# Attention with two mixture layers on one core: block means of the last units turned a slot sooner, and the order of step 1 around its normalisation changed

## The chip, the core and the metric

The kernel runs on one core of one Trainium2 chip. The metric is the device time of one execution in microseconds. Before the change three executions took 823.92, 826.63 and 828.28 us; the median is 826.63 us.

## What is computed

The program has three stages in a row, all in 32-bit floating point. Two sequences of 768 tokens with 8 heads of 64 features go through an attention in which a query sees the 31 keys around it and 24 block summaries (the maximum of a block's 32 keys, the mean of its 32 values). The result, 1536 tokens of 512 features, goes through a mixture of four experts and then through one wide layer.

```python
def _attn_ref(q, k, v):
    k_sum = k.reshape(B, H, nb, block, D).max(axis=3)
    v_sum = v.reshape(B, H, nb, block, D).mean(axis=3)
    scores_l = scale * np.matmul(q, k.transpose(0, 1, 3, 2))      # masked to |i - j| < 16
    scores_s = scale * np.einsum('bhsd,bhnd->bhsn', q, k_sum) + np.log(block)
    a = softmax(concatenate([scores_l_m, scores_s]))
    return np.matmul(a, concatenate([v, v_sum], axis=2))

def _moe_ref(x, domain_probs, w1, w2):
    p = domain_probs / (domain_probs.sum(-1, keepdims=True) + 1e-09)
    for e in range(4):
        out += p[:, e:e + 1] * (np.maximum(x @ w1[e], 0.0) @ w2[e])

def _moe2_ref(x, w_in, w_out):
    h = x @ w_in
    return (h * (1.0 / (1.0 + np.exp(-1.702 * h)))) @ w_out
```

## The kernel before

**Attention in slots.** The attention is cut into 8 units (one sequence, two heads) of 3 groups k. Units 0 to 3, groups 0 to 11, run in a software pipeline of 18 slots in which each engine does one stage of several groups: TensorE the scores of group slot-1, VectorE the mask, ScalarE the exponentials, VectorE the inverted sums (`invert_sums`), GpSimd the normalisation (`normalize`), TensorE the transposes, VectorE or ScalarE the copy of the transposed weights, TensorE the values, ScalarE the copy into `xa` (`take_x`). Units 4 to 7 are spread over the steps behind.

**Block means and maxima.** For each unit VectorE sums the blocks of values (`value_sums`, `v_sum`), TensorE turns the sums (`turn_value_sums`, line L1628), ScalarE scales them (`value_means`, L958) and GpSimd spreads them over the value windows (`spread_value_means`, L708). VectorE takes the maxima of the keys (`key_maxima`, L1271) and GpSimd spreads them (`spread_key_maxima`, L690). Unit 4 (named `KT` in the code) has its maxima taken at the end of the slots and its values summed in step 1.

**Steps.** The mixtures are 48 steps g. A step holds one pair of blocks of hidden features; its first matrix product is made by seven half-size products P1 to P7 (a Strassen scheme, order P1, P2, P5, P6, P7, P4, P3), and the second one by eight pieces `down(g, t)`. Each number is split in a high and a low part, so that a product is three matmuls (L1651, L1652, L1653). Step 0 has four plain tiles instead (`first_tile`), which start as soon as the blocks of `xa` are split: ScalarE makes the high parts (`high_moved`), VectorE the low parts (`low_moved`, L1348).

**Weights.** The weights of a step come by one 1 MB transfer into `stage[g % 2]`. GpSimd makes four sums (`sum_weights`, L719 to L725), the low parts of what came (`low_raw`, L730) and of the sums (`low_sums`, L736), and those of the second matrix (`low_down`, L742; for step 0 `low_first`, L752 and L758). ScalarE makes the high parts (`high_raw`, L982; `high_sums`; `high_down`). On step g TensorE weaves the products of step g with `down(g - 1, t)`. Behind product P6 ScalarE keeps a copy of a bank (`keep(g, 1)`, L1024), for which P7 waits.

**Orders.** All orders are written out by hand, one instruction stream for each engine, and every engine works its own in order. SyncE issues all transfers from one list. In its list the values of unit 5 stand behind a wait for unit 4's `value_sums`, since both use the same buffer, and behind them come the value windows of unit 5, two stores of split weights of step 1 and the load of `stage` for step 3:

```python
def load_value_columns(u):
    if u >= KT:
        sp.wait_ge(vsum_done, u)
    sp.dma_start(v_cols[values_at(u)][:], v_t[u, :, :])
```

Of the kernel before, what the change touches and what calls it, by code (L numbers as in the profile page):

```python
# [19 lines left out]
KT = DM // P  # L20
# [7 lines left out]
B_GROUPS = KT * GROUPS  # L28
# [37 lines left out]


B12, T2 = 7, 3
MADE_0 = (0, B12, 6, 2, 1, 3, 4, 5)

READY_0 = {"C12": 1, "C22": 2, "C11": 3, "C21": 4}

# [47 lines left out]
def attention_moe_ffn(nc, consts, q_t, k_w, v_t, v_w, probs, weights, p_rows, split, out):  # L120
    ctx = ExitStack()
    with ctx:
# [174 lines left out]
        def values_due(slot, lag):  # L297


            return [u for u in range(KT) if slot - lag == GROUPS * u + L_SUM + (u > 0)]  # L300
# [381 lines left out]
        def _(pool):  # L682
# [44 lines left out]
            def low_raw(g):  # L727

                pool.wait_ge(rawhi_done, own(g))
                nc.gpsimd.tensor_tensor(wu_lo[:, g % 2, 0:RAW], stage[:, g % 2, 0:RAW],  # L730
                                        wu_hi[:, g % 2, 0:RAW].bitcast(F32), ALU.subtract).then_inc(rawlo_done, 1)
# [13 lines left out]
            def low_first(n):  # L745

                half = slice(RAW // 2 * (n % 2), RAW // 2 * (n % 2 + 1))
                if n < 2:
                    pool.wait_ge(rawhi_done, 1)
                    if n == 1:  # L750
                        pool.wait_ge(rawlo_first, 1)
                    nc.gpsimd.tensor_tensor(wu_lo[:, 0, half], stage[:, 0, half], wu_hi[:, 0, half].bitcast(F32),  # L752
                                            ALU.subtract).then_inc(rawlo_first if n == 0 else rawlo_done, 1)
                else:
                    pool.wait_ge(dnhi_done, 2)
                    if n == 3:
                        pool.wait_ge(dnlo_first, 1)
                    nc.gpsimd.tensor_tensor(wd_lo[:, 0, half], stage[:, 0, 4 * BW:][:, half],  # L758
                                            wd_hi[:, 0, half].bitcast(F32),
                                            ALU.subtract).then_inc(dnlo_first if n == 2 else dnlo_done, 1)  # L760
# [74 lines left out]
            for slot in range(SLOTS):  # L835
                for k in group(slot, L_NORM):
                    normalize(k)
                for u in keys_due(slot):
                    spread_key_maxima(u)
                for u in values_due(slot, 2):  # L840
                    if u:
                        spread_value_means(u, norm_done, slot - L_NORM + 1)
                    else:
                        spread_value_means(u, kwin_done, 2)
                if slot in (11, 12):
                    low_first(slot - 11)

            for g in range(STEPS):
                ph, part = preparing(g)
# [15 lines left out]
                if more:  # L865
                    sum_weights(g + 1)
                    if g == 0:
                        spread_key_maxima(KT)
                    low_raw(g + 1)
                for k in step_group(g):  # L870
                    normalize(k)
                if ph == 2 and part == 0:

                    sum_moved(ph, 1)
                    low_down(g)
                    low_moved(ph, 0)
                    low_moved(ph, 2)
                    sum_moved(ph, 2)
                    low_moved(ph, 1)
                    low_down(g + 1)  # L880
                    continue
# [60 lines left out]
        def _(act):  # L942
# [24 lines left out]
            def take_x(k):  # L967

                act.wait_ge(pv_done, k + 1)
                nc.scalar.activation(columns(k), x_bank(k)[:, 0:GT * QT], ACT.Copy).then_inc(x_done, 1)  # L970
# [119 lines left out]
            for slot in range(SLOTS):  # L1090
                for k in group(slot, L_X):
                    take_x(k)
                for k in group(slot, L_EXP):
                    exponent(k)
                for k in group(slot, L_TRANS):
                    if on_act(k):
                        copy_prob_t(k)
                for u in values_due(slot, 1):
                    value_means(u)
                if slot == 10:  # L1100
                    high_raw(0)
                if slot == 12:
                    high_moved(0, 0)
                if slot == 13:
                    high_moved(0, B12)
                if slot == 14:
                    high_down(0, 0)
                    high_down(0, 1)
                if slot == 16:
                    high_moved(0, 6)  # L1110
                    high_moved(0, 2)
            high_moved(0, 1)
            high_raw(1)
            high_sums(1)
            high_hidden(0, "C12")
# [148 lines left out]
        def _(dve):  # L1264
# [165 lines left out]
            for slot in range(SLOTS):  # L1430
                if slot == 0:
                    key_maxima(0)
                for k in group(slot, L_EXP):
                    mask_scores(k)
                for k in group(slot, L_NORM):
                    invert_sums(k)
                for k in group(slot, L_TRANS):
                    if not on_act(k):
                        copy_prob_t(k)
                for u in keys_due(slot):  # L1440
                    key_maxima(u)
                for u in values_due(slot, 0):
                    value_sums(u)
                if slot == 1:
                    normalize_weights()
                if slot == 13:
                    low_moved(0)
                if slot == 14:
                    low_moved(B12)
                    sum_first(1)  # L1450
                if slot == 15:
                    key_maxima(KT)
            low_moved(6)
            low_moved(2)
            low_moved(1)
            gate(0, "C12")
            gate(0, "C22")
            low_hidden(0, "C12")
# [11 lines left out]
            for g in range(1, STEPS):  # L1470
                if g == 1:

                    add_c11(1)
                    mask_scores(B_GROUPS)
                    gate(1, "C11")
                    take_y(0, 0)
                    value_sums(KT)
                    take_y(0, 1)
                    low_hidden(1, "C11")
                    invert_sums(B_GROUPS)  # L1480
                    take_y(0, 2)
                    low_moved(5)
                    take_y(0, 3)
                elif second(g):
                    if paired(g - 3):
                        take_product(g - 3, "P4", 1)
# [102 lines left out]
        def _(pe):  # L1589
# [170 lines left out]
            for slot in range(SLOTS):  # L1760
                for k in group(slot, L_SCORE):
                    scores(k)
                for k in group(slot, L_TRANS):
                    transpose(k)
                for k in group(slot, L_VAL):
                    values(k)
                for u in values_due(slot, 1):
                    turn_value_sums(u)
            pe.wait_ge(rawlo_done, 1)
            pe.wait_ge(vmean_done, KT)  # L1770
            pe.wait_ge(xlo_dve, low_parts(0, 0))
# [20 lines left out]
            product(1, "P7")  # L1792
            down(0, 2)
            down(0, 3)
            turn_value_sums(KT)
            down(0, 4)
            down(0, 5)
            transpose(B_GROUPS)
            product(1, "P4")
            down(0, 6)  # L1800
# [113 lines left out]
```

## Time and profile before

| | |
|---|---|
| median of three executions | 826.63 us |
| lowest, highest | 823.92, 828.28 us |
| profiled execution, its own time | 824.39 us |
| its span (first to last instruction) | 822.2 us |
| granted TensorE clock, mean share | 0.998 |
| TensorE busy | 798.7 us, 97% |
| VectorE, ScalarE, GpSimd busy | 69%, 52%, 71% |

The profiled execution lies 2.24 us under the median; 2.2 us of its time lie outside the span. TensorE is nearly always busy, so the table says that only its gaps and its own work make the time; where those gaps are, the rows below tell.

### The profile page before, as it was taken

To read this page: it belongs to the slowest core of one execution; us is meant where nothing else is said; L and a number is where in the kernel's file an instruction comes from. 1 tells how busy PE (TensorE), PEld (TensorE's weight loads), DVE (VectorE), ACT (ScalarE), POOL (GpSimd) and SP (SyncE) were. 2 spreads that over 40 slices of the span, in tenths; PEclk is the share of its full clock that TensorE was granted. 3 is DMA by queue.
4 is the path that set the end of the run, shared out by engine and by line. 5 is a ranking of instruction groups with operands and counts; after the bars stand their busy time and mean duration, and the time that the engine had idled before them with its cause. 6 is when DMAs were issued, how large, how long until landed. Compare 5 with 4: busy or idle time off the path is not lost.

```text
span 822.2 us, 14168 instructions
## 1 busy us (share of the span) xinstructions
PE 798.7 (97%) x4894; PEld 779.6 (95%) x4894; DVE 568.6 (69%) x1194; ACT 427.8 (52%) x943; POOL 580.8 (71%) x406
## 2 busy tenths in 40 slices
PE   5889999999999999999999999999999999999997
PEld 4778999999999999999999999999999999999997
DVE  5888656666665566687877877665666665677777
ACT  3865445445445454546545544434456553656663
POOL 3697765655666699678778685777488873588794
PEclk9999999999999999999999999999999999999999
DMA  9959547375444354446245343343544445373412
GB/s 265 285 122 338 214 196 235 141 262 216 159 179 175 141 214 161 171 155 232 104 184 198 122 198 142 142 189 143 217 160 187 175 172 205 104 293 143 165 66 77
DMA packets 39957, 148.92 MB, mean 181 GB/s; under 512 B 16208, under 2 KB 17360, under 8 KB 36688
## 3 DMA queue, kind: packets, MB, share of 16 engines
q1 hardware_dynamic: 39888, 148.03, 49.9%
q8 instruction: 39, 0.64, 0.3%
q14 instruction: 30, 0.25, 0.1%
HBM read 100.81 MB, written 47.21 MB: 180 GB/s over the span
## 4 chain that ended last, share of the span: by engine, by line
PE 76%; POOL 10%; issue 5%; ACT 4%; DVE 3%; DMA 1%; SPq 0%; ACTq 0%; DVEq 0%; POOLq 0%
PE bank L1651 25%; PE bank L1653 24%; PE bank L1652 24%; POOL wd_lo L809 2%; POOL h_raw L832 2%; POOL t_raw L832 2%; PE bank L1606 2%; ACT prob L949 1%; PE bank L1617 1%; PE bank L1643 1%; DMA v_cols<-v_t 1%; ACT xb_first_hi L1050 1%; POOL wu_lo L730 1%; POOL wd_lo L742 1%; ACT xb_last_hi L1074 0%
## 5 line engine op out<-in xcount | busy, mean ns | idle before, releaser
L1358 DVE TENSOR_TENSOR xa<-bank,xa 128x384 f32<-128x384 f32 x208 | 115.8, 556 | 136.7 <-PE bank L1653 133.9
L1651 PE MATMUL bank<-h_hi,wd_hi 128*128 128x384 f32 x448 | 150.5, 336 | 0.3 <-DVE xa L1356 0.2
L1653 PE MATMUL bank<-h_lo,wd_hi 128*128 128x384 f32 x448 | 149.8, 334 | 0.0
L1652 PE MATMUL bank<-h_hi,wd_lo 128*128 128x384 f32 x448 | 149.7, 334 | 0.0
L1040 ACT ACTIVATE h_hi<-bank 128x384 fp32r<-128x384 f32 x112 | 55.1, 492 | 136.9 <-DVE bank L1415 113.5
L742 POOL TENSOR_TENSOR wd_lo<-stage,wd_hi 128x1024 fp32r<-128x1024 f32 x27 | 65.2, 2413 | 82.9 <-ACT wd_hi L997 82.8
L809 POOL TENSOR_TENSOR wd_lo<-stage,wd_hi 128x512 fp32r<-128x512 f32 x60 | 85.9, 1437 | 40.2 <-ACT wd_hi L1087 39.5
L1651 PE MATMUL bank<-xb_other_hi,wu_hi 128*128 128x384 f32 x336 | 113.0, 336 | 0.8 <-ACT snap L1024 0.2
L1653 PE MATMUL bank<-xb_other_lo,wu_hi 128*128 128x384 f32 x336 | 112.3, 334 | 0.0
L1652 PE MATMUL bank<-xb_other_hi,wu_lo 128*128 128x384 f32 x336 | 112.3, 334 | 0.0
L1024 ACT ACTIVATE snap<-bank 128x384 f32<-128x384 f32 x141 | 69.2, 491 | 64.0 <-PE bank L1653 63.1
L1651 PEld LDWEIGHTS bank<-h_hi,wd_hi 128*128 128x128 f32 x448 | 84.1, 188 | 2.3 <-DVE xa L1356 1.1
L1652 PEld LDWEIGHTS bank<-h_hi,wd_lo 128*128 128x128 f32 x448 | 84.1, 188 | 0.0
L1653 PEld LDWEIGHTS bank<-h_lo,wd_hi 128*128 128x128 f32 x448 | 84.1, 188 | 0.0
L1415 DVE SCALAR_TENSOR_TENSOR bank<-bank,p_bc 128x384 f32<-128x384 f32 x128 | 71.5, 559 | 10.4 <-PE bank L1653 9.5
L1370 DVE TENSOR_TENSOR xa<-bank,xa 128x384 f32<-128x384 f32 x124 | 66.7, 548 | 14.5 <-PE bank L1653 13.5
L1065 ACT ACTIVATE h_raw<-bank 128x384 f32<-128x384 f32 x80 | 39.3, 492 | 70.2 <-DVE bank L1415 45.7
L1651 PE MATMUL bank<-xb_first_hi,wu_hi 128*128 128x384 f32 x196 | 68.2, 348 | 0.0
L1651 PEld LDWEIGHTS bank<-xb_other_hi,wu_hi 128*128 128x128 f32 x336 | 63.0, 188 | 2.9 <-ACT snap L1024 2.7
L1652 PE MATMUL bank<-xb_first_hi,wu_lo 128*128 128x384 f32 x196 | 65.7, 335 | 0.0
L1653 PE MATMUL bank<-xb_first_lo,wu_hi 128*128 128x384 f32 x196 | 65.7, 335 | 0.0
L1652 PEld LDWEIGHTS bank<-xb_other_hi,wu_lo 128*128 128x128 f32 x336 | 63.1, 188 | 0.0
(120 smaller groups left out, 2078.7 us busy)
## 6 DMA issues: line engine op xcount, KB each, us to landing
stage<-weights SPq DMA_DIRECT2D x25, 1024.0 KB, 4.9
split<-wu_hi SPq DMA_DIRECT2D x24, 896.0 KB, 3.6
split<-wu_lo SPq DMA_DIRECT2D x24, 896.0 KB, 5.6
wu_hi<-split SPq DMA_DIRECT2D x23, 896.0 KB, 6.3
wu_lo<-split SPq DMA_DIRECT2D x23, 896.0 KB, 8.0
stage<-weights SPq DMA_DIRECT2D x23, 512.0 KB, 4.5
k_win<-k_w SPq DMA_DIRECT2D x8, 720.0 KB, 8.1
v_win<-v_w SPq DMA_DIRECT2D x8, 576.0 KB, 9.3
```

The costliest lines, as they stand in the source:

```text
L742: nc.gpsimd.tensor_tensor(wd_lo[:, g % NWD, :], stage[:, g % 2, 4 * BW:], wd_hi[:, g % NWD, :].bitcast(F32), ALU.subtract).then_inc(dnlo_d ...
L809: nc.gpsimd.tensor_tensor(lo.rearrange("p (f n) -> p f n", f=2), held_source(name), hi.bitcast(F32).rearrange("p (f n) -> p f n", f=2), AL ...
L832: nc.gpsimd.tensor_tensor(hidden_sum(n), a, b, ALU.subtract).then_inc(tsum_done, 1)
L1024: nc.scalar.activation(snap[:, n, :], ps_x(g), ACT.Copy).then_inc(snap_done, 1)
L1040: nc.scalar.activation(h_hi[:, g % 2, TILE[c], :], hidden(g, c), ACT.Copy).then_inc(hhi_done, 1)
L1065: nc.scalar.activation(hidden_raw(g, c), hidden(g, c), ACT.Copy).then_inc(raw_done, 1)
L1358: nc.vector.tensor_tensor(at, y_bank(g, t), at, ALU.add).then_inc(y_taken, 1)
L1370: nc.vector.tensor_tensor(at, source, at, ALU.add).then_inc(y_taken, 1)
L1415: nc.vector.scalar_tensor_tensor(hidden(g, c), hidden(g, c), 0.0, p_bc[:, q % 2, tokens(half)], ALU.max, ALU.mult).then_inc(gated_done, 1)
L1651: nc.tensor.matmul(dst, w_h, a_h, start=first, stop=False, skip_group_check=True)
L1652: nc.tensor.matmul(dst, w_l, a_h, start=False, stop=False, skip_group_check=True)
L1653: return nc.tensor.matmul(dst, w_h, a_l, start=False, stop=last, skip_group_check=True)
```

## The change

No operation is added or taken away. Orders change in three places.

In the slots the block means of units 1 to 3 are turned, scaled and spread earlier within their slot (TensorE turns them ahead of the transposes, ScalarE scales them ahead of the exponentials) and GpSimd spreads them one slot sooner; the second half of step 0's first low parts (`low_first`) goes one slot later in exchange.

Behind the slots the split of block 1 (`high_moved(0, 1)`, `low_moved(1)`) goes ahead of block 2's, and VectorE takes the key maxima of unit 4 behind these two low parts instead of ahead of them.

In step 1 GpSimd normalises group 12 ahead of `low_raw(2)`, VectorE copies the banks of `down(0, t)` (`take_y`) sooner, and `value_sums(KT)`, `low_moved(5)` and `low_hidden(1, "C11")` stand behind four of these copies; TensorE turns the sums of unit 4 two pieces later.

```diff
-MADE_0 = (0, B12, 6, 2, 1, 3, 4, 5)
+MADE_0 = (0, B12, 6, 1, 2, 3, 4, 5)
...
-                for u in values_due(slot, 2):
+                for u in values_due(slot, 1):
                     if u:
                         spread_value_means(u, norm_done, slot - L_NORM + 1)
-                    else:
+                for u in values_due(slot, 2):
+                    if u == 0:
                         spread_value_means(u, kwin_done, 2)
-                if slot in (11, 12):
-                    low_first(slot - 11)
+                if slot in (11, 13):
+                    low_first(slot // 12)
...
-                    low_raw(g + 1)
+                    if g > 1:
+                        low_raw(g + 1)
                 for k in step_group(g):
                     normalize(k)
+                if g <= 1:
+                    low_raw(g + 1)
...
-                if slot == 15:
-                    key_maxima(KT)
             low_moved(6)
+            low_moved(1)
+            key_maxima(KT)
             low_moved(2)
-            low_moved(1)
...
                     add_c11(1)
+                    take_y(0, 0)
                     mask_scores(B_GROUPS)
                     gate(1, "C11")
-                    take_y(0, 0)
+                    take_y(0, 1)
+                    take_y(0, 2)
+                    invert_sums(B_GROUPS)
+                    take_y(0, 3)
                     value_sums(KT)
-                    take_y(0, 1)
+                    low_moved(5)
                     low_hidden(1, "C11")
-                    invert_sums(B_GROUPS)
-                    take_y(0, 2)
-                    low_moved(5)
-                    take_y(0, 3)
...
             down(0, 3)
-            turn_value_sums(KT)
             down(0, 4)
             down(0, 5)
+            turn_value_sums(KT)
             transpose(B_GROUPS)
```

VectorE behind the slots, before: the rows run from the first low part (block 0) to the first gates of step 0; `xb_..._lo` are the low parts, `xa<-xa` a sum of blocks, `k_max` the maxima of unit 4.

```order
L1309 COPY prob_t<-bank 120x512
L1348 TENSOR_TENSOR xb_first_lo<-xa,xb_first_hi 128x768
L1342 TENSOR_TENSOR xa<-xa 128x768
L1271 TENSOR_REDUCE k_max<-k_win 128x24
L1348 TENSOR_TENSOR xb_last_lo<-xa,xb_last_hi 128x768
L1348 TENSOR_TENSOR xb_first_lo<-xa,xb_first_hi 128x768 x2
```

The same place of the changed kernel (its lines are numbered 8 higher on VectorE):

```order
L1317 COPY prob_t<-bank 120x512
L1356 TENSOR_TENSOR xb_first_lo<-xa,xb_first_hi 128x768
L1350 TENSOR_TENSOR xa<-xa 128x768
L1356 TENSOR_TENSOR xb_last_lo<-xa,xb_last_hi 128x768
L1356 TENSOR_TENSOR xb_first_lo<-xa,xb_first_hi 128x768
L1279 TENSOR_REDUCE k_max<-k_win 128x24
L1356 TENSOR_TENSOR xb_first_lo<-xa,xb_first_hi 128x768
```

The maxima moved behind two low parts of 128x768 each.

VectorE in step 1, before, from the gate of tile C11 on; `xa<-bank` are the copies `take_y`, `v_sum` the sums of unit 4's values, `row_sum_e` and `row_inv` the inverted sums of group 12, `h_lo` is `low_hidden(1, "C11")`.

```order
L1415 SCALAR_TENSOR_TENSOR bank<-bank,p_bc 128x384
L1356 COPY xa<-bank 128x384
L1278 TENSOR_REDUCE v_sum<-v_cols 128x24
L1356 COPY xa<-bank 128x384
L1425 TENSOR_TENSOR h_lo<-bank,h_hi 128x384
L1300 TENSOR_SCALAR row_sum_e<-row_sum 128x4
L1303 RECIPROCAL row_inv<-row_sum_e 128x4
L1356 COPY xa<-bank 128x384
L1348 TENSOR_TENSOR xb_last_lo<-xa,xb_last_hi 128x768
L1356 COPY xa<-bank 128x384 x2
L1395 TENSOR_TENSOR bank<-bank,snap 128x384
```

The same place of the changed kernel; its first copy stands now ahead of the mask rows, which are above this piece.

```order
L1423 SCALAR_TENSOR_TENSOR bank<-bank,p_bc 128x384
L1364 COPY xa<-bank 128x384 x2
L1308 TENSOR_SCALAR row_sum_e<-row_sum 128x4
L1311 RECIPROCAL row_inv<-row_sum_e 128x4
L1364 COPY xa<-bank 128x384
L1286 TENSOR_REDUCE v_sum<-v_cols 128x24
L1356 TENSOR_TENSOR xb_last_lo<-xa,xb_last_hi 128x768
L1433 TENSOR_TENSOR h_lo<-bank,h_hi 128x384
L1364 COPY xa<-bank 128x384
L1403 TENSOR_TENSOR bank<-bank,snap 128x384
```

The sums of unit 4's values stand behind the fourth copy instead of the first.

GpSimd in step 1, before: the last of the four weight sums of step 2, the low parts, the normalisation of group 12 (`prob`), the low parts of the sums and the spread means of unit 4.

```order
L725 TENSOR_TENSOR w_sum<-stage,w_sum 128x256
L730 TENSOR_TENSOR wu_lo<-stage,wu_hi 128x1024
L698 TENSOR_TENSOR prob<-prob,row_inv 128x480
L736 TENSOR_TENSOR wu_lo<-w_sum,wu_hi 128x768
L708 COPY v_win<-v_mean 24x1536
```

The same place of the changed kernel:

```order
L725 TENSOR_TENSOR w_sum<-stage,w_sum 128x256
L698 TENSOR_TENSOR prob<-prob,row_inv 128x480
L730 TENSOR_TENSOR wu_lo<-stage,wu_hi 128x1024
L736 TENSOR_TENSOR wu_lo<-w_sum,wu_hi 128x768
L708 COPY v_win<-v_mean 24x1536
```

The normalisation and the 1024-wide low part changed places; the four weight sums stay ahead of both. SyncE's list of transfers is the same in both kernels.

## Rows read from the trace of the kernel before

**Rows 1.** The page's head and its first part.

```profile
span 822.2 us, 14168 instructions
PE 798.7 (97%) x4894; PEld 779.6 (95%) x4894; DVE 568.6 (69%) x1194; ACT 427.8 (52%) x943; POOL 580.8 (71%) x406
```

**Rows 2.** Waits of TensorE: us in total, times, longest.

```profile
PE bank L1617 <- POOL prob L698: 3.1, 3, 1.4
PE bank L1643 <- POOL v_win L708: 2.4, 2, 1.7
```

**Rows 3.** Windows: us, each engine's busy time, granted TensorE clock, DMA share, GB/s.

```profile
44.00:48.00 4.00, 1.82 (x24) 1.31 (x24) 3.93 (x5) 3.10 (x9) 3.62 (x3) 0.98 1.20 269
48.00:51.00 3.00, 3.00 (x36) 2.78 (x36) 2.88 (x4) 2.29 (x4) 2.83 (x3) 0.50 1.02 243
72.00:75.00 3.00, 1.60 (x9) 1.28 (x10) 2.02 (x4) 0.66 (x2) 3.00 (x3) 1.00 0.97 354
```

**Rows 4.** Timeline of VectorE behind the slots: start, us, instruction, idle before.

```profile
49.51 0.94 DVE L1271 TENSOR_REDUCE k_max<-k_win 128x24 f32<-128x768 f32 x1
50.56 1.23 DVE L1348 TENSOR_TENSOR xb_last_lo<-xa,xb_last_hi 128x768 fp32r<-128x768 f32 x1
```

**Rows 5.** Timeline of GpSimd behind the slots.

```profile
52.34 1.16 POOL L690 COPY k_win<-k_max 128x288 f32<-128x288 f32 x1
...
58.34 3.45 POOL L758 TENSOR_TENSOR wd_lo<-stage,wd_hi 128x512 fp32r<-128x512 f32 x2
```

**Rows 6.** Timeline of TensorE in step 1.

```profile
63.04 0.33 PE L1651 MATMUL bank<-h_hi,wd_hi 128*128 128x384 f32 x1
...
66.16 0.33 PE L1651 MATMUL bank<-xb_last_hi,wu_hi 128*128 128x384 f32 x1
...
70.05 0.40 PE L1628 MATMUL bank<-cst,v_sum 128*24 128x128 f32 x2
...
74.67 0.65 PE L1617 MATMUL bank<-cst,prob 128*120 128x128 f32 x4 [1.40 <-POOL prob L698]
75.08 0.42 PE L1651 MATMUL bank<-xb_last_hi,wu_hi 128*128 128x384 f32 x1
```

**Rows 7.** Timeline of VectorE in step 1.

```profile
67.35 0.93 DVE L1278 TENSOR_REDUCE v_sum<-v_cols 128x24 f32<-128x768 f32 x1
```

**Rows 8.** Timeline of GpSimd in step 1.

```profile
67.44 0.75 POOL L719 TENSOR_TENSOR w_sum<-stage 128x256 f32<-128x256 f32 x1
...
70.57 3.10 POOL L730 TENSOR_TENSOR wu_lo<-stage,wu_hi 128x1024 fp32r<-128x1024 f32 x1
73.64 0.98 POOL L698 TENSOR_TENSOR prob<-prob,row_inv 128x480 f32<-128x480 f32 x1
```

**Rows 9.** SyncE's queue: its wait, two issues of `stage`, the second one's landing.

```profile
SPq L567 <- DVE v_sum L1278: 3.9, 1, 3.9
...
61.82 0.33 SPq L583 DMA_DIRECT2D stage<-weights  x1
...
70.11 0.66 SPq L583 DMA_DIRECT2D stage<-weights  x1
...
stage<-weights SPq DMA_DIRECT2D x1, 1024.0 KB, 12.2
```

**Rows 10.** Timelines of GpSimd, ScalarE and TensorE in step 2.

```profile
82.43 0.74 POOL L719 TENSOR_TENSOR w_sum<-stage 128x256 f32<-128x256 f32 x1 [0.86 <-DMA stage<-weights]
...
84.01 1.06 ACT L982 ACTIVATE wu_hi<-stage 128x1024 fp32r<-128x1024 f32 x1 [2.54 <-POOL stage L721]
85.65 0.49 ACT L1040 ACTIVATE h_hi<-bank 128x384 fp32r<-128x384 f32 x1 [0.58 <-DVE bank L1415]
...
88.52 0.49 ACT L1024 ACTIVATE snap<-bank 128x384 f32<-128x384 f32 x1 [0.60 <-PE bank L1653]
...
89.37 0.33 PE L1651 MATMUL bank<-xb_last_hi,wu_hi 128*128 128x384 f32 x1
```

**Rows 11.** Windows, while `stage` for step 3 is under way.

```profile
75.00:82.00 7.00, 7.00 (x45) 7.00 (x44) 4.80 (x9) 2.89 (x6) 5.26 (x3) 1.00 1.01 420
```

More of the change, by code:

```diff
@@ L1092, in _ @@
                     take_x(k)
+                for u in values_due(slot, 1):
+                    if u:
+                        value_means(u)
                 for k in group(slot, L_EXP):
@@ L1098, in _ @@
                 for u in values_due(slot, 1):
-                    value_means(u)
+                    if u == 0:
+                        value_means(u)
                 if slot == 10:
@@ L1110, in _ @@
                     high_moved(0, 6)
-                    high_moved(0, 2)
             high_moved(0, 1)
+            high_moved(0, 2)
             high_raw(1)
@@ L1762, in _ @@
                     scores(k)
+                for u in values_due(slot, 1):
+                    if u:
+                        turn_value_sums(u)
                 for k in group(slot, L_TRANS):
@@ L1767, in _ @@
                 for u in values_due(slot, 1):
-                    turn_value_sums(u)
+                    if u == 0:
+                        turn_value_sums(u)
             pe.wait_ge(rawlo_done, 1)
```

## The prediction

> **What bounds the kernel now.** I read the page's head first: TensorE is busy 97% of the span [rows 1], so a change of order pays only where TensorE stands still, and only if nothing else comes late in its place. The waits of TensorE show where it stands still at all: 3.1 us in three waits for the normalised weights and 2.4 us in two for spread block means [rows 2]. All that the diff touches runs before 80 us. I then read the timelines of every engine from 36 to 100 us, SyncE's queue with them. Two stretches stand out. The first is the tail of the slots, where TensorE is busy 1.82 of the 4 us from 44 to 48 us, and after which its granted clock is 0.50 (1.2 GHz) from 48 to 51 us [rows 3]. The second is step 1. From product P7 at 66.16 us to P4 at 75.08 us pass 8.92 us [rows 6]. A product or a piece of `down` takes 1.04 us (three of them lie between 63.04 and 66.16), so P7 and four pieces are 5.2 us; with 0.35 for the turned sums and 0.41 for the transposes (74.67 to 75.08) the work is 5.96 us. The rest, 2.96 us, is waiting: 1.4 us for the normalisation [rows 6] and the remainder in four short waits for bank copies and round the turn. From about 76 us on, TensorE waits for nothing until past 100 us.
>
> **The change part by part.** It adds and removes no instruction; each term is a wait that goes or comes.
>
> Slots. With the means of unit 3 spread one slot sooner, the wait for them (1.7 us, the longer of [rows 2]) has no cause. What is late next is the last normalisation: GpSimd now has the 512-wide low part where the spread stood, and ahead of it the same VectorE work. I take the last values as 0.3 to 1.0 us earlier. If the clock stays at 2.4 GHz, about 1.5 us of the 3 us at half clock come back too [rows 3]. So TensorE enters step 0 with a lead of 0.3 to 2.5 us.
>
> That lead is capped by GpSimd. Its chain after the last normalisation is weight sums, key maxima of unit 4, low parts; it reaches the maxima at 52.34 us and ends with step 0's second matrix at 58.34 + 3.45 = 61.79 us [rows 5], and `down(0, 0)`, at 63.04 us [rows 6], needs that. VectorE now takes the maxima behind two low parts of 1.2 to 1.3 us (one is 1.23 in [rows 4]). If these start a microsecond sooner than 50.56, at 49.6, the maxima end at 49.6 + 2.5 + 0.9 = 53.0 us: GpSimd waits some 0.6 us for them, and regains about that, since its next piece no longer runs beside VectorE's low parts. I leave its end at 61.8 us, between 61.2 and 62.6. So `down(0, 0)` comes at 61.9 us, a lead of at most 1.1 us.
>
> Step 1. With the copies sooner, the short waits go. The normalisation follows the four weight sums instead of standing behind `low_raw`, so it starts at 70.57 rather than 73.64 us [rows 8]; these sums can begin up to 0.6 us sooner, since their `stage`, issued at 61.82 [rows 9], was there before GpSimd was free at 67.44. Normalised weights at 71.0 us, transposes 0.41: P4 at 71.5 us instead of 75.08, a lead of 3.6 us (3.0 if the sums don't move). `low_raw(2)` ends at 71.0 + 3.1 = 74.1 us; product P1 of step 2 needs it at 75.7: hidden. `low_moved(5)`, moved down, ends about 70.8 us, also in time. If the story ended here, the gain would be 3.6 us.
>
> The queue behind `v_sum`. It doesn't end here. SyncE stands 3.9 us on unit 4's `v_sum` [rows 9], which ended at 67.35 + 0.93 = 68.28 us [rows 7]. Queued behind it are the values and value windows of unit 5, two stores and the load of `stage` for step 3, issued at 70.11 us and landed 12.2 us later [rows 9]. The diff puts `v_sum` behind the fourth copy. That copy waits for `down(0, 3)`, which ends at 61.9 + 6 x 1.04 = 68.15 us (six pieces from `down(0, 0)`); then come the inverted sums' tail and the copy, to 68.9 us, and `v_sum`, to 69.8 us: 1.5 us later than now although TensorE is ahead. (With no lead at `down(0, 0)` it is 70.9 us, 2.6 later; with 1.7 us of lead 69.2, 0.9 later.) The transfers are never idle in that stretch (share 1.01 at 420 GB/s [rows 11]), and part of the delay is covered by the query loads that are still under way; what is not is a hole that everything behind inherits. I take 1.1 us of the 1.5, with 0 (all covered) and 2.6 (nothing covered, no lead) as ends. `stage` for step 3 is then usable at 82.43 + 1.1 = 83.5 us.
>
> What waits for it. GpSimd had to wait 0.86 us for this landing already, and ScalarE stood 2.54 us before `high_raw(3)` at 84.01 us, 1.58 us behind the landing [rows 10]. Behind `high_raw(3)` ScalarE has, in order, the high part of a hidden tile, the exponentials of group 13, a `take_x` and `keep(2, 1)`, for which P7 of step 2 waits. From 84.01 to 88.52 are 4.51 us, of which 0.58 and 0.60 are idle [rows 10]; the work is 3.33 us, with the 0.49 of `keep` 3.82. So P7 can't start before landing + 1.58 + 3.82 = landing + 5.4 us. Now that is 87.8 us, and P7 starts at 89.37 us [rows 10]: 1.5 us of slack, seen nowhere among the waits. A lead of 3.6 us would put P7 at 85.8; with the landing unmoved it waits until 87.8 and keeps 1.5 us, with the landing at 83.5 it waits until 88.9 and keeps 0.5 us. At the ends of the hole (0 and 2.6 us) the change is a gain of 1.5 or a loss of 1.1 us. GpSimd's low parts for step 3 and all later steps have more room than that, so what P7 keeps is the result.
>
> A rule on the queue: the Trainium skill, page "DMA: Bandwidth & Descriptors", section "Queues, rings and completion order", says that on each of the 16 transfer engines descriptors are consumed in ring order. By it nothing behind the late issue can overtake and the whole 1.5 us would pass on wherever the ring runs empty; the trace agrees so far as `stage`, last of the list, takes 12.2 us to land [rows 9]. By that the gain would be 0.1 instead of 0.5 us.
>
> **The sum.** Profiled execution: 824.39 - 0.5 = 823.9 us. It lies 2.2 us under the median of the runs shown; I forecast against that median: 826.63 - 0.5 = 826.1 us.
>
> **The rivals.**
> 1. The clock falls (slower than before, by one mechanism). TensorE would stand about 3 us before P7 of step 2, from 85.8 to 88.9 us. The one fall in the trace came after 44 to 48 us, with 1.82 us busy of 4; after 72 to 75 us, 1.60 busy of 3, the clock stayed [rows 3]. A gap of 3 us is emptier than both. Three microseconds at 1.2 instead of 2.4 GHz cost 1.5 us: net 1.0 us slower, 827.6 us. It decides once the fall costs over 0.5 us. The Trainium skill, "TensorE: Matmul & The Clock Gate", "Part 1: The HAM clock gate", says that the clock knows two states only and that its observation is free-running, so that equal kernels differ from run to run; this is why I give a chance and no yes or no. Chance 0.27.
> 2. `stage` for step 3 doesn't matter (it lands by 80.4 us, or ScalarE is quicker through its list): step 1's whole 3.6 us stay, 823.0 us. For it speaks only that the waits show nothing at P7; against it the 12.2 us to landing. Chance 0.14.
> 3. More than 4.1 us faster: rival 2, and GpSimd's chain ends early too, so that the lead of the slots (up to 2.5 us) adds: 821 us. Chance 0.07.
> 4. `v_sum` or the maxima come later than worked out and the fall comes as well: 1.1 + 1.5 us or more slower, 829 us; over 4.1 us in few cases. Chance 0.09.
> The forecast (a gain of 0.5, between -1.1 and 1.5 us) has 0.43.
>
> **How the numbers follow.** The range must hold rivals 1 and 2 and leave out most of 3 and the far end of 4: 822.8 to 828.8 us; the forecast's own is 825.1 to 827.7. 0.5% of 826.63 us are 4.1 us, about what a measurement of this kernel can tell from no change. Faster than that: rival 3 and a little for the scatter of the runs, 0.10; slower: half of rival 4 and scatter, 0.07; within: 0.83.
>
> **What would show it.** In the changed profile I expect no wait for `v_win` in the tail, normalisation 12 near 70 us, P4 of step 1 near 71.5 us, SyncE's wait for `v_sum` some 1.5 us longer, `stage` for step 3 landing at 83 to 84 us, and a new wait of TensorE of 2 to 3 us for `snap` (L1024's counterpart) before the second P7, perhaps with clock 0.5 behind it. I am wrong if that wait isn't there, or if `stage` lands before 81 us; then the time is nearer 823.

## The result and the profile after

| | before | changed |
|---|---|---|
| median of 20 runs each, same chip, us | 824.96 (823.3 to 829.14) | 827.55 (824.27 to 830.93) |
| ratio, 95% interval | | 1.0029 [1.0018, 1.004] |
| profiled execution, us | 824.39 | 826.53 |

The changed kernel is slower by 0.29%, 2.4 us of 824.96 (1.5 to 3.3 by the interval). That lies within the 0.5% to which I gave 0.83, and the predicted 826.1 us is inside the spread of its runs. But the forecast was 0.5 us faster and the kernel is 2.4 us slower: the sign was wrong. The time itself came out near 826.1 us partly by luck: I had counted from the median of three executions, 826.63 us, and that of twenty is 824.96 us, 1.67 us lower. The head of the changed page shows TensorE 1.2 us busier than in [rows 1] with as many instructions, and 0.7 us more idle:

```profile
span 824.1 us, 14168 instructions
PE 799.9 (97%) x4894; PEld 780.1 (95%) x4894; DVE 570.7 (69%) x1194; ACT 427.4 (52%) x943; POOL 580.0 (70%) x406
```

The waits of TensorE (columns as in [rows 2]) show the exchange. The waits for `v_win` are gone, and one of 3.3 us for `snap` stands there; before, the waits for `snap` came to 0.2 us in total:

```profile
PE bank L1624 <- POOL prob L698: 3.5, 5, 1.6
PE bank L1658 <- ACT snap L1028: 3.5, 2, 3.3
PE bank L1635 <- DVE v_sum L1286: 1.7, 2, 0.9
```

Step 1 as TensorE sees it (timeline: start, us, instruction; compare [rows 6]). `down(0, 0)` begins at 61.46 us, the four transposes at 70.94 and P4 at 71.76:

```profile
61.46 0.33 PE L1658 MATMUL bank<-h_hi,wd_hi 128*128 128x384 f32 x1
...
70.94 0.65 PE L1624 MATMUL bank<-cst,prob 128*120 128x128 f32 x4
...
71.76 0.44 PE L1658 MATMUL bank<-xb_last_hi,wu_hi 128*128 128x384 f32 x1 [0.16 <-DVE xb_last_lo L1356]
```

VectorE and GpSimd, their timelines, in the same stretch (compare [rows 7] and [rows 8]). `v_sum` ends at 69.09 + 0.94 = 70.03 us, 1.75 later than the 68.28 of before; the normalisation is 3.74 us sooner:

```profile
69.09 0.94 DVE L1286 TENSOR_REDUCE v_sum<-v_cols 128x24 f32<-128x768 f32 x1
```

```profile
66.77 0.73 POOL L719 TENSOR_TENSOR w_sum<-stage 128x256 f32<-128x256 f32 x1
...
69.90 0.99 POOL L698 TENSOR_TENSOR prob<-prob,row_inv 128x480 f32<-128x480 f32 x1
...
84.36 0.75 POOL L719 TENSOR_TENSOR w_sum<-stage 128x256 f32<-128x256 f32 x1 [4.59 <-DMA stage<-weights]
```

The last of these is GpSimd's first use of the `stage` for step 3, at 82.43 us in [rows 10]: 1.93 us later. SyncE's queue releases the next `v_cols` as soon as `v_sum` has ended, and `stage` behind it:

```profile
70.06 0.33 SPq L567 DMA_DIRECT2D v_cols<-v_t  x1
...
72.63 1.68 SPq L583 DMA_DIRECT2D stage<-weights  x1
```

Then ScalarE, which now waits 7.76 us where it waited 2.54 [rows 10], and P7 of step 2 on TensorE:

```profile
85.96 1.06 ACT L986 ACTIVATE wu_hi<-stage 128x1024 fp32r<-128x1024 f32 x1 [7.76 <-POOL stage L721]
...
89.07 0.47 ACT L1028 ACTIVATE snap<-bank 128x384 f32<-128x384 f32 x1
...
89.60 0.45 PE L1658 MATMUL bank<-xb_last_hi,wu_hi 128*128 128x384 f32 x1 [3.26 <-ACT snap L1028]
```

And the windows round it (columns as in [rows 3]): TensorE is busy 0.34 of 3 us, and in the stretch from 90 us on its granted clock is near 0.5, the 1.2 GHz level:

```profile
86.00:89.00 3.00, 0.34 (x2) 0.01 (x1) 1.09 (x3) 3.00 (x11) 2.92 (x3) 1.00 1.00 424
90.00:93.00 3.00, 3.00 (x12) 2.17 (x11) 0.08 (x1) 1.04 (x3) 2.78 (x3) 0.54 0.04 11
```

The transfers show where the delay begins. Windows from 66 to 74 us, the kernel before first, then the changed one: the DMA share falls from 1.07 and 0.98 to 0.74 and 0.65, so the transfer engines run partly empty while the queue stands behind `v_sum`.

```profile
66.00:70.00 4.00, 3.88 (x20) 3.04 (x19) 3.96 (x14) 3.48 (x11) 3.76 (x5) 1.00 1.07 310
70.00:74.00 4.00, 3.05 (x15) 2.12 (x14) 3.62 (x8) 1.70 (x4) 4.00 (x3) 1.00 0.98 287
```

```profile
66.00:70.00 4.00, 4.00 (x24) 3.73 (x23) 3.70 (x12) 3.69 (x12) 3.77 (x6) 1.00 0.74 225
70.00:74.00 4.00, 3.84 (x23) 3.12 (x22) 4.00 (x8) 1.47 (x4) 4.00 (x3) 1.00 0.65 150
```

Laid end to end, in starts of TensorE's instructions of the two profiles. "First tile" is the first tile of step 0, "P1" the first product of step 3:

| stretch | before, us | changed, us | difference |
|---|---|---|---|
| start of the span to first tile | 50.01 | 48.82 | -1.19 |
| first tile to `down(0, 0)` | 13.03 | 12.64 | -0.39 |
| `down(0, 0)` to P4 of step 1 | 12.04 | 10.30 | -1.74 |
| P4 of step 1 to P7 of step 2 | 14.29 | 17.84 | +3.55 |
| P7 of step 2 to P1 of step 3 | 8.30 | 9.91 | +1.61 |
| P1 of step 3 to P1 of step 4 | 17.78 | 17.78 | 0 |
| the rest | 706.7 | 706.8 | +0.1 |

All of the lead, 3.32 us, is won before 72 us and given back with 5.16 us between 72 and 100 us. Of the lead 0.55 us lie before TensorE's first instruction (7.00 against 7.55 us) and are no work of the change. Behind that the kernels are equal: in all profiles of this study the rest is 706.6 to 707.2 us.

### The profile page after: what moved, and what is told of

Same layout as the page of the kernel before. It is cut to its first block, busy times and chain, and to the rows that moved or that the text cites. A ratio compares the mean times of both kernels' runs of the same rounds, so it can differ in the third digit from the quotient of the medians.

```text
span 824.1 us, 14168 instructions
## 1 busy us (share of the span) xinstructions
PE 799.9 (97%) x4894; PEld 780.1 (95%) x4894; DVE 570.7 (69%) x1194; ACT 427.4 (52%) x943; POOL 580.0 (70%) x406
## 4 chain that ended last, share of the span: by engine, by line
PE 76%; POOL 8%; issue 5%; DVE 5%; ACT 3%; DMA 2%; SPq 1%; ACTq 0%; DVEq 0%; POOLq 0%
PE bank L1658 25%; PE bank L1660 24%; PE bank L1659 24%; POOL wd_lo L809 2%; POOL h_raw L832 2%; POOL t_raw L832 2%; PE bank L1613 1%; DMA stage<-weights 1%; PE bank L1624 1%; PE bank L1650 1%; DMA v_cols<-v_t 1%; DVE masked L1298 1%; ACT xb_first_hi L1054 1%; DVE row_sum_e L1308 1%; DVE v_sum L1286 0%
```

## The experiments

Three sets of four kernels (e, g, h) ran, each set beside its own runs of the kernel before: 7 to 13 executions of each kernel, 30 to 35 of the kernel before. The sets e and g had one chip, h another. Each result gives the median and the ratio to the kernel before with its 95% interval.

### e1 and h4: the changed kernel with `v_sum` at its old place

```diff
                     gate(1, "C11")
+                    value_sums(KT)
                     take_y(0, 1)
...
                     take_y(0, 3)
-                    value_sums(KT)
```

Expected of e1: 

> The changed kernel with the sums of unit 4's values (value_sums(KT)) put back behind the gate of tile C11, ahead of the second copy; all else as changed. My theory (the late stage for step 3 takes the gain back): SyncE's wait for v_sum ends near 67.6 us instead of 70.0, stage for step 3 is used by GpSimd near 82 us instead of 84.36, and P7 of step 2 starts near 87.5 us instead of 89.60, so the profiled span is 1.5 to 2.5 us shorter than that of the changed kernel. Rival A (the loss sits in the slots or behind them, not in v_sum's place): P7 comes earlier by less than 0.5 us. Rival B (the clock's fall alone makes the loss): P7 comes earlier, but the wait before it is still over 1.5 us, the clock still falls in part of the executions, and the median stays within 1 us of the changed kernel's.

Expected of h4, the same kernel once more: 

> The changed kernel with v_sum back behind the gate of C11 (e1_vsum_early) once more, since that profile came from an execution that began late. My theory: SyncE's wait for v_sum ends near 67.5 us, P7 of step 2 follows P4 after 15.5 to 16.5 us (14.3 without a wait, 17.84 in the changed kernel), with a wait of 1 to 2 us. If it follows after 14.3 us without a wait again, v_sum's place alone makes the whole wait.

Measured: e1 823.9 us, 0.9997 [0.9978, 1.0017]; h4 823.58 us, 0.9978 [0.9964, 0.9992]. The slots of e1's profiled execution took 7.5 us longer, which says nothing of the change, so I read h4's. Of the two, h4 is faster than the kernel before, and e1 can't be told from it; both lie below the changed kernel (1.0018 to 1.004). SyncE's queue, then GpSimd and TensorE:

```profile
68.33 0.33 SPq L567 DMA_DIRECT2D v_cols<-v_t  x1
```

```profile
82.28 0.73 POOL L719 TENSOR_TENSOR w_sum<-stage 128x256 f32<-128x256 f32 x1 [1.85 <-DMA stage<-weights]
```

```profile
68.82 0.44 PE L1658 MATMUL bank<-h_hi,wd_hi 128*128 128x384 f32 x1 [0.81 <-DVE xa L1364]
...
87.50 0.45 PE L1658 MATMUL bank<-xb_last_hi,wu_hi 128*128 128x384 f32 x1 [0.17 <-ACT snap L1028]
```

With one instruction moved back, `stage` is usable 2.1 us sooner than in the changed kernel and the wait shrinks from 3.26 to 0.17 us; the clock doesn't fall. The price is a wait of 0.81 us in step 1 for the bank copy that now stands behind `v_sum`. From P4 of step 1 to P7 of step 2 are 14.62 us, against 17.84 in the changed kernel; I had expected 15.5 to 16.5 and a wait of 1 to 2 us. The place of `v_sum` is the cause of the loss.

### e2 and e3: the load of `stage` for step 3 ahead of the queue

```diff
             for u in (KT, KT + 1):
...
                 load_queries(u)
+                if u > KT:
+                    load_weights(3)
...
                 for x in weights_due(g):
-                    load_weights(x)
+                    if g:
+                        load_weights(x)
```

e2 is the changed kernel with it, e3 the kernel before with it. Expected of e2: 

> The changed kernel; in SyncE's list the load of stage for step 3 stands ahead of the values and value windows of unit 5 and of the two stores of step 1's split weights, so that it no longer waits for v_sum. My theory: stage lands near 73 us, GpSimd's sums for step 3 no longer wait, P7 of step 2 starts near 86 us without a wait, the clock stays up there, and the whole lead of step 1 (3.6 us) is kept: about 3.5 us less than before, 5 to 6 us less than the changed kernel. Rival A: the transfers are the bound whatever their order (the stores land late instead, high_raw(3) waits for them or product P5 for its values): no gain over the changed kernel, or under 2 us. Rival B: the lead is lost later on anyway: a gain at P7 that is gone by 200 us.

Expected of e3: 

> The kernel before, with the same change of SyncE's list alone. My theory: there P7 of step 2 had 1.5 us of slack behind this transfer, so nothing moves: within 0.7 us of the kernel before. Rival: the transfer's order is worth something by itself (then e2's gain isn't that of the lead kept): over 1.5 us faster.

Measured: e2 822.57 us, 0.9974 [0.9958, 0.999]; e3 824.97 us, 0.9989 [0.9971, 1.0007]. In e2's queue `stage` is issued before `v_sum` matters, and `v_cols` at 71.35 us delays nobody:

```profile
68.09 0.33 SPq L583 DMA_DIRECT2D stage<-weights  x1
...
71.35 0.33 SPq L567 DMA_DIRECT2D v_cols<-v_t  x1
```

The waits of TensorE from 60 to 100 us are then this one row:

```profile
PE bank L1661 <- DVE xb_last_lo L1359: 0.2, 1, 0.2
```

From P4 of step 1 to P7 of step 2 are 14.39 us in e2 and 14.30 in e3, against 14.29 before and 17.84 in the changed kernel. So nothing but the landing of this `stage` holds P7. The gain is smaller than expected: about 3.5 us less than before was the forecast for e2, 2.1 us (0.26%) by the ratio is what came, and P7 of step 2 starts 1.95 us sooner than before (87.42 against 89.37). The kernel before, in which P7 did not wait, gets nothing from the earlier load that the runs can tell; the changed one gains 0.5%.

### e4: 14 more multiplications in the wait

```diff
+                if g == 2:
+                    pe.wait_ge(probt_done, B_GROUPS + 1)
+                    for _ in range(14):
+                        nc.tensor.matmul(bank[6][:, 0:HALF], wu_hi[:, 0, 0:P], xb_first[0][:, 0, 0, :], ...)
                 product(g, "P7")
```

The changed kernel; their product goes to a bank that P7 overwrites. Expected: 

> The changed kernel with 14 extra matmuls of 128x384 (2.4 us) into a bank that nobody reads then, between down(1, 3) and P7 of step 2, where TensorE waited 3.26 us; the result is unchanged by them. They end ahead of what P7 waits for. If the fall of the clock behind that wait costs what I think (about 1.7 us in an execution that shows it), the granted clock stays 1.0 from 86 to 100 us and the median is 1 to 1.7 us less than the changed kernel's, P7 still at 89.6 us. If the fall costs little, the median stays within 0.4 us; if the matmuls are themselves in the way, it is longer.

Measured: 825.64 us, 1.0001 [0.9988, 1.0014], beside 1.0029 for the changed kernel: work was added, and the time fell. The timeline of TensorE and the window behind it:

```profile
90.50 2.59 PE L1866 MATMUL bank<-xb_first_hi,wu_hi 128*128 128x384 f32 x14
94.06 0.44 PE L1658 MATMUL bank<-xb_last_hi,wu_hi 128*128 128x384 f32 x1 [0.97 <-ACT snap L1028]
```

```profile
94.00:98.00 4.00, 3.94 (x22) 3.44 (x23) 1.53 (x4) 1.51 (x4) 3.62 (x4) 1.00 0.03 12
```

P7 still starts 5.22 us behind GpSimd's use of `stage` (88.84 us here, since this execution too was late in the slots), but the clock stays at 2.4 GHz there. From P7 to P4 of step 2 are 4.16 us, 4.04 before, 5.64 in the changed kernel. So the fall costs 1.5 us in the profile; the medians differ by 1.9 us, the ratios by 2.3.

### g1 and g2: two of the three parts of the change alone

g1 is the kernel before with the part in the slots alone (the order of `spread_value_means`, `value_means` and `turn_value_sums`, and the second half of `low_first` a slot later), g2 with step 1's (`low_raw` behind `normalize`, the VectorE list, the turn). The part behind the slots (block 1 ahead of block 2, the key maxima behind the two low parts) is in neither, and no run has it alone. Expected of g1: 

> The kernel before with the change in the slots alone (means of units 1 to 3 turned, scaled and spread sooner, second half of step 0's low parts a slot later); the key maxima, block 2 and step 1 as before. By my reading of the changed profile this part brings some 0.5 to 1 us at the first tile of step 0; P7 of step 2 then still has its slack, so the gain stays: 0 to 1 us faster than before. Rival (the slots part is what makes the changed kernel slow): over 1 us slower.

Expected of g2: 

> The kernel before with the change in step 1 alone (normalisation ahead of the low parts, copies sooner, v_sum behind the fourth copy, sums turned later). My theory: this part alone carries the loss. P4 follows down(0, 0) after about 10 us instead of 12.04, SyncE's issue behind v_sum comes 1 to 2.5 us later, and P7 of step 2 follows P4 after 16 to 18 us instead of 14.29: no gain, 0 to 3 us slower than before by whether the clock falls. Rival (the loss needs all parts): 1 to 2 us faster than before.

Measured: g1 825.2 us, 1.0003 [0.9986, 1.002]; g2 827.65 us, 1.0022 [1.0004, 1.0039]. The slots' part moves nothing that the runs can tell, and neither do the profiles settle it: from TensorE's first instruction to the first tile are 41.9 us in g1 and h3 and 41.82 in the changed kernel, but 42.4 to 43.5 in h4, e2, h1 and g4, which have the same slots (h1 with its extra work; the late executions of e4 and e1 have 45.5 and 48.6), and 42.1 to 42.5 in the five profiles of the old slots (before, e3, g2, g3, h2). Step 1's part alone brings a loss of the size of the whole change's. g2's SyncE queue, GpSimd, TensorE and the window behind P7:

```profile
71.12 0.33 SPq L567 DMA_DIRECT2D v_cols<-v_t  x1
```

```profile
85.62 0.74 POOL L719 TENSOR_TENSOR w_sum<-stage 128x256 f32<-128x256 f32 x1 [5.11 <-DMA stage<-weights]
```

```profile
90.83 0.69 PE L1654 MATMUL bank<-xb_last_hi,wu_hi 128*128 128x384 f32 x1 [3.76 <-ACT snap L1027]
```

```profile
94.00:98.00 4.00, 4.00 (x18) 3.96 (x18) 1.47 (x3) 0.00 (x0) 1.62 (x2) 0.62 0.77 315
```

### g3 and g4: step 1's part with `stage` first, and both cures at once

g3 is g2 with e2's edit, g4 the changed kernel with the edits of e1 and e2. Expected of g3: 

> The kernel before with the change in step 1 and with the load of stage for step 3 ahead of unit 5's values in SyncE's list; slots and key maxima as before. My theory: the 1.7 to 3 us of step 1 are kept, P7 follows P4 after 14.3 us: 1.7 to 3 us faster than before. If the slots part brings something of its own, this is slower than e2_stage_first (0.9974 of before) by 0.5 to 1 us; if the slots part costs, it is faster than that one.

Expected of g4: 

> The changed kernel with both mends: stage for step 3 first in SyncE's list and v_sum back behind the gate of C11. If the order of the transfers is all that cost, v_sum's place no longer matters and this is within 0.7 us of e2_stage_first (0.9974 of before). If a late v_sum costs something else as well, it is 1 us or more faster than that; if an early v_sum holds up the copies that TensorE waits for, it is up to 1 us slower.

Measured: g3 823.63 us, 0.9988 [0.9968, 1.0007]; g4 823.06 us, 0.9973 [0.9959, 0.9986]. Against g2 the medians differ by 4.0 us, the ratios by 2.8; the two intervals still touch between 1.0004 and 1.0007, and g3 itself, forecast 1.7 to 3 us faster than before, can't be told from it. Whether the slots' part adds to it (g3 against e2) can't be told: the intervals overlap. Nor does moving `v_sum` add to `stage` first (g4 against e2): one cure is enough.

### h2: `v_sum` late, and nothing else

```diff
-                    value_sums(KT)
                     take_y(0, 1)
...
                     take_y(0, 3)
+                    value_sums(KT)
...
-            turn_value_sums(KT)
             down(0, 4)
             down(0, 5)
+            turn_value_sums(KT)
```

The kernel before with that. Expected: 

> The kernel before with one thing changed: value_sums(KT) behind the fourth copy and the turn of these sums behind down(0, 5). No lead is won in step 1, P4 stays where it is. By the chain landing + 5.4 us with 1.5 us of slack: SyncE's issue comes 3 to 4 us later, the landing 2 to 4 us later, P7 of step 2 waits 0.5 to 2.5 us: 0.5 to 2.5 us slower than before, a little more where the clock falls. Rival (only the lead makes the wait): no wait at P7, within 0.4 us of before.

Measured: 828.21 us, 1.004 [1.0022, 1.0057], as slow as the changed kernel run again (h3, below), with no lead won and none to give back. GpSimd, ScalarE and TensorE in its profile:

```profile
84.86 0.73 POOL L719 TENSOR_TENSOR w_sum<-stage 128x256 f32<-128x256 f32 x1 [3.21 <-DMA stage<-weights]
```

```profile
86.44 1.06 ACT L982 ACTIVATE wu_hi<-stage 128x1024 fp32r<-128x1024 f32 x1 [4.47 <-POOL stage L721]
...
89.55 0.48 ACT L1024 ACTIVATE snap<-bank 128x384 f32<-128x384 f32 x1
```

```profile
73.59 0.93 PE L1617 MATMUL bank<-cst,prob 128*120 128x128 f32 x4 [1.76 <-POOL prob L698]
...
90.08 0.45 PE L1651 MATMUL bank<-xb_last_hi,wu_hi 128*128 128x384 f32 x1
```

```profile
74.00:78.00 4.00, 4.00 (x17) 4.00 (x16) 0.62 (x2) 0.92 (x3) 2.78 (x2) 0.59 0.88 274
```

`v_cols` is issued at 71.02 us, `stage` used 13.84 us later, and P7 follows 5.22 us behind it, at 90.08: ScalarE works without a gap from 86.44 us to the end of `snap` at 89.55 + 0.48 = 90.03 us. Counted from `down(0, 0)`, `stage` is used 3.48 us later than before and P7 comes 1.76 us later (28.09 against 26.33 us): the slack of 1.7 us is used up and the rest is the loss.

There is also a second fall of the clock that I had not expected, from 74 us on behind the wait for the normalised weights: P4 to P1 of step 2 takes 5.66 us there, 4.25 before. In this profile it costs nothing more, since P7 could not have started sooner than `snap` allowed; without the fall TensorE would have waited some 1.4 us longer in front of P7. The late landing explains the 1.76 us by itself. The profiled execution is the fastest of the twelve (825.42 us), so what the other eleven consist of it doesn't show.

### h1 and h3: the tail of the slots filled, and the changed kernel again

```diff
             for slot in range(SLOTS):
...
+                if slot in (14, 15, 16):
+                    if slot == 14:
+                        pe.wait_ge(rawhi_done, 1)
+                    for _ in range({14: 8, 15: 5, 16: 3}[slot]):
+                        nc.tensor.matmul(bank[3][:, 0:HALF], wu_hi[:, 0, 0:P], wu_hi[:, 0, 0:HALF], ...)
```

h1 is g4 with these 16 extra multiplications, h3 the changed kernel itself. Expected of h1: 

> The kernel with both mends (stage for step 3 first, v_sum early) and with 8, 5 and 3 extra matmuls of 128x384 into a bank that is free then, ahead of the transposes of slots 14 and 15 and of the values of slot 16, where TensorE waits; the result is unchanged by them. In every profile so far the clock is at half for 3.4 or 6.8 us at the end of the slots. If that fall sets the first tile's time, the clock stays at 1.0 and the median is 1 to 2 us less than that of the kernel with both mends (0.9973 of before). If GpSimd's chain caps TensorE's lead behind the slots (down(0, 0) needs step 0's low parts), TensorE waits for them instead and the median stays within 0.5 us.

Expected of h3: 

> The changed kernel itself, once more, on the chip of the other three. My theory: about 1.003 of before; P7 of step 2 waits 2.5 to 4 us for snap. The granted clock behind that wait is 0.5 for 3.4 or 6.8 us in this profile as well, if the length of the gap decides it; if it depends on the execution, it may stay at 1.0.

Measured: h1 822.38 us, 0.9964 [0.9946, 0.9981]; h3 827.73 us, 1.0039 [1.0019, 1.0059], so the loss repeats. h3 has the changed kernel's profile: `v_cols` issued at 70.19, `stage` used at 84.45, P7 at 89.68 behind a wait of 3.20 us.

In h1 the clock stays at 2.4 GHz through the tail, in which every other profile has 3.4 to 6.8 us at half of it. The first tile comes at 50.13 us, hardly sooner than the 50.47 of g4:

```profile
47.60 0.65 PE L1627 MATMUL bank<-cst,prob 128*120 128x128 f32 x4 [0.93 <-POOL prob L701]
...
50.13 0.45 PE L1661 MATMUL bank<-xb_first_hi,wu_hi 128*128 128x384 f32 x1
```

In g4, at half the clock, the same transposes start at 47.52 us:

```profile
47.52 1.11 PE L1627 MATMUL bank<-cst,prob 128*120 128x128 f32 x4 [1.99 <-POOL prob L701]
```

Both wait for GpSimd's normalisation: the tail is bound by that chain, at either clock. h1 against g4 is 0.9964 against 0.9973, on two chips and with intervals that overlap; the gain isn't settled. h1 has the lowest ratio of all, and its interval and those of g4, e2 and h4 lie under 1 and below that of the changed kernel.

## Why the prediction was right and wrong, by its steps

Two terms failed: the part of the late issue that I took as covered (0.4 of 1.5 us), and the fall of the clock, which the sum had at nothing. They are told below as "the hole" and "the clock".

**The slots: right in size, and in part by luck.** No wait for the spread means is left, and the first tile is 1.19 us sooner, of which 0.55 are the start of the execution. The clock didn't stay up: it is at half for 6.8 us, from 42 us on, where before it was for 3.4 us:

```profile
40.00:44.00 4.00, 2.37 (x30) 1.72 (x30) 3.97 (x9) 3.98 (x15) 3.61 (x3) 0.80 0.97 261
44.00:48.00 4.00, 2.91 (x40) 2.39 (x38) 3.96 (x5) 1.81 (x4) 3.60 (x4) 0.50 1.21 261
```

The lead at `down(0, 0)` was to be 1.1 us, at 61.9; it came at 61.46, 1.58 us sooner. I had called GpSimd's chain the cap. It ended at 57.86 + 3.26 = 61.12 us, and TensorE had no gap in front of `down(0, 0)`, so the cap didn't bind:

```profile
52.67 1.09 POOL L690 COPY k_win<-k_max 128x288 f32<-128x288 f32 x1 [1.74 <-DVE k_max L1279]
53.72 2.38 POOL L730 TENSOR_TENSOR wu_lo<-stage,wu_hi 128x1024 fp32r<-128x1024 f32 x1
...
57.86 3.26 POOL L758 TENSOR_TENSOR wd_lo<-stage,wd_hi 128x512 fp32r<-128x512 f32 x2
```

The wait for the maxima was 1.74 us, not 0.6, and yet the chain ended sooner. What I had argued for this, that GpSimd's next piece no longer runs beside VectorE's low parts, shows in that piece: 2.38 us, against 3.11 in the kernel before, where VectorE's low parts lasted until 54.31 us:

```profile
53.46 3.11 POOL L730 TENSOR_TENSOR wu_lo<-stage,wu_hi 128x1024 fp32r<-128x1024 f32 x1
```

What the slots' part is worth by itself isn't measurable in g1.

**Step 1: right at P4.** Normalisation at 69.90 (about 70 predicted), P4 at 71.76 (71.5), lead 3.32 us at P4 (3.6), the 0.55 us of the start among them. From `down(0, 0)` to P4 the change saved 1.74 us where the forecast had 2.5 (3.6 - 1.1); the larger lead at `down(0, 0)` made up for most of it.

**The late `v_sum`: right.** 70.03 us (69.8), 1.75 us later (1.5).

**The hole: the first step that failed.** I wrote that "part of the delay is covered by the query loads that are still under way" and took 1.1 us of the 1.5. Nothing is covered. From SyncE's issue of `v_cols` to GpSimd's use of `stage` it is nearly the same time whenever the issue comes (e1 and e4 were late as whole executions):

| kernel | `v_cols` issued, us | `stage` used, us | between |
|---|---|---|---|
| g1 | 67.54 | 81.27 | 13.73 |
| before | 68.31 | 82.43 | 14.12 |
| h4 | 68.33 | 82.28 | 13.95 |
| changed | 70.06 | 84.36 | 14.30 |
| h3 | 70.19 | 84.45 | 14.26 |
| h2 | 71.02 | 84.86 | 13.84 |
| g2 | 71.12 | 85.62 | 14.50 |
| e4 | 74.39 | 88.84 | 14.45 |
| e1 | 76.45 | 89.86 | 13.41 |

13.4 to 14.5 us over 8.9 us of difference in the issue, 3.6 of them without e1 and e4. 1.75 us at the issue became 1.93 us at the landing, where the forecast had 1.1: 0.25 of the difference is `v_sum` itself, the rest the cover that wasn't there. The share of 1.01 in [rows 11] says that the transfers are busy from 75 us on; at the moment at which the issue is late, from 66 to 74 us, the share is 0.74 and 0.65, and with `v_sum` back at its place (h4) 1.07 and 1.01. The rule that I weighed against my own reading (the Trainium skill, "DMA: Bandwidth & Descriptors", "Queues, rings and completion order") gave the whole delay, and these rows agree with it.

**What P7 waits for: right.** "Landing + 5.4 us" is 5.2 us: 84.36 to 89.60 in the changed kernel, and 5.21 to 5.23 in h3, g2, h2, e4 and h4 (in e1, where P7 waited for nothing, 5.44). With the use of `stage` at 84.36 the step gives 89.8 us where 89.60 is measured. The slack of 1.5 us that no view of waits shows was real: it is 89.37 - (82.43 + 5.22) = 1.7 us.

**The sum without the clock** is then 89.60 - 89.37 = +0.23 us where I had -0.5: 0.7 us of the error are the hole, and with them the gain is gone. Counted from TensorE's first instruction, without the 0.55 us of the start, it is 82.60 - 81.82 = +0.78 us.

**The clock: the second step that failed, the larger error, and a choice.** I gave the fall 0.27 in rival 1 and a part in rival 4, and 0.43 to a forecast without it. The wait of 3.26 us was at the upper end of the 2 to 3 us that I forecast, and the fall came in all three profiles with a wait of over 3 us (changed, h3, g2), and not in e4, where the wait was filled. Rival 1 was to cost 1.5 us; the profile has 9.91 - 8.30 = 1.61. It is rival 1, with the larger hole, that happened: +0.23 + 1.61 = +1.84 of the 1.9 us by which the spans differ. That rival and the forecast stood at different sides of zero, so I let the sign hang on this one chance; with the hole as it was, both would have come out on the slow side. I had put the gap as "emptier than both" in [rows 3], and no row gave the fall less ground than the forecast. Rival 1's 827.6 us lies beside the measured 827.55 by luck: its +1.0 us stands on a median that was 1.67 us too high.

**What stays open.** The medians differ by 2.4 us and the profiled executions by 2.1; the difference is inside the interval. Whether the clock falls behind the wait in each execution of the changed kernel can't be seen, since only profiled ones show the place of a fall. The mean granted clock of every execution is on record, though. It is 0.9920 over the 32 executions of the changed kernel, none above 0.996, and 0.9945 over the 30 of the kernel before beside h3; 0.0025 of 825 us are 2.1 us, an estimate of the most that the lower clock can account for. The tail of the slots is in it too, where the two profiles of the changed kernel have 6.8 us at half the clock and the kernel before 3.4; e2 and h4, at 0.9933, are faster than before all the same. h2's twelve executions have 0.9917, its profiled one 0.996; how the 3.0 us by which its median is longer divide between the delay of P7 and the clock is open. Open is also what the part behind the slots does alone.

## What to carry to other kernels

A consumer without a wait in the profile may be a microsecond from having one. Work out its slack (here: use of `stage` + 5.2 us against the start of P7) for each transfer queued behind an instruction that you move, and add the delay of the issue to the landing in full. Where a lead turns into one long wait of TensorE, count the clock with it: 3.3 us of waiting cost 1.6 us more. Here the urgent load issued earlier, or the moved instruction put back, took the loss away and in e2, g4 and h4 left a gain of 0.2 to 0.3%, and even useless multiplications in the gap brought the ratio back to 1.

## What the runs showed of the hardware

- Adding 14 multiplications (2.59 us of TensorE) in a wait of 3.3 us brought the ratio from 1.0029 to 1.0001; the fall of the clock behind the empty wait costs 1.6 us (9.91 against 8.30 us for the same work), in g2 2.8 us (11.14).
- The clock also fell behind 70 to 74 us of h2, where TensorE was busy 2.24 of the 4 us with one wait of 1.76 us in it, while in the kernel before it stayed after 1.60 of 3 us [rows 3]. Of two similar stretches one brought a fall and the other didn't:

```profile
70.00:74.00 4.00, 2.24 (x13) 1.53 (x12) 2.95 (x6) 1.98 (x4) 4.00 (x4) 0.98 0.52 118
```

- The time from a delayed issue to the use of the last load behind it stayed between 13.4 and 14.5 us in nine profiles.
- GpSimd's 128x1024 subtraction `low_raw(1)` took 2.38 to 2.40 us in the eight profiles in which it starts behind VectorE's low parts (changed, e1, e2, e4, g4, h1, h3, h4), and 2.84 to 3.11 us in the six in which it starts beside them (before, e3, g1, g2, g3, h2).
